# Attention followed by two feed-forward layers in float32: the values of two heads side by side in column halves of the array, their sums by ones in its quarters, and the rotary step on GpSimd

## The chip, the core and the metric

One core of a Trainium2 chip runs the whole program. The metric is the time of one execution on the device, in microseconds. Engines are named as the profile names them: PE (TensorE), PEld (its weight loads), DVE (VectorE), ACT (ScalarE), POOL (GpSimd), SP (the queue that issues every DMA).

## The reference

q, k and v are float32 of 4 batches x 8 heads x 576 positions x 64. Cut to what matters:

```
q_rot, k_rot = (rotate(q), rotate(k))            # x1*cos - x2*sin, x1*sin + x2*cos
scores = scale * np.matmul(q_rot, k_rot.transpose(0, 1, 3, 2))
scores = scores - np.max(scores, axis=-1, keepdims=True)
attn = np.exp(scores)
attn = attn / (np.sum(attn, axis=-1, keepdims=True) + 1e-09)
x = np.matmul(attn, v)                           # then [2304 tokens, 512]
h = x @ w_in;  x = (h - np.tanh(h)) @ w_out      # d_ff = 2048
h = x @ w_in2; x = (h * sigmoid(1.702 * h)) @ w_out2
```

## The kernel before

There are 32 heads in 16 pairs, and a head's 576 positions are 5 tiles of 128 (the last holds 64). The order of all work is written out by hand, engine by engine; semaphores tie the engines together.

For each head the program does this. **Rotary** (`rope`, on DVE, three products and sums over 128 partitions x 576 for the keys of a pair and three for its queries). **Split** into a high and a low part of float32 (`keys_hi` and `queries_hi` on ACT, `keys_lo` and `queries_lo` on DVE), with a DMA copy of the high part to the other 64 partitions (`copy_k`, `copy_q`). **Near scores** (`near_scores`, entry "M" of the ring, L414): two matmuls of 288 columns for a tile of 128 queries, from which DVE takes the rows' maxima (`row_max`, L667). **Maxima across** (`maxima_across`, "R", L421): PE transposes the 5 columns of maxima, and DVE puts them into the rows of the query tile (`place_maxima`, L674). **Scores** (`scores`, "S", L431 and L437): four matmuls for a tile of 128 keys, with the maximum subtracted inside the product, and the exponential on ACT (`exp`, L537). **Values** (`probs_v`, L449): two float32 matmuls of 288 columns with 128 x 128 weights, in which 64 columns are V and 64 columns are ones, so that the sums of the exponentials come out beside the values. ACT copies the result out (`copy_pv`), the sums go through DMA, a reciprocal on DVE (`invert`), a scratch in HBM and a broadcast DMA, and POOL multiplies (`normalise`, L382).

PSUM has 3 slots of two banks for S, M and R, which go round in the order of the list `RING`; an entry waits until the entry 3 places before it has been read. The last two banks belong to the values. PE issues, in a head, S and the values of two tiles before, with the near scores of the next head between them:

```
for t in range(TILES):
    ...
    if now:
        scores(h, t)
    if now and g >= 0:
        probs_v(g)
    if ahead and t < 2:
        near_scores(h + 1, 2 * t + 1)
        near_scores(h + 1, 2 * t + 2)
```

Keys and queries have 4 sets of tiles (`k_hl`, `k_one`, `q_hh`, `q_max`), and are split 3 heads ahead. After the heads come the two feed-forward layers (L485, L500, L503); from head 17 on, the first x tiles and weights for them are cut into high and low parts between the heads' work (`early_x`, `early_w`).

## Time and profile before

| | |
|---|---|
| median of 3 runs | 1146.83 us (1146.66 to 1147.7) |
| the profiled execution | 1147.27 us, of which the span is 1145.5 us |
| PE busy | 1104.1 us, 96% of the span |
| DVE busy | 552.4 us, 48% |
| ACT busy | 425.7 us, 37% |
| POOL busy | 57.1 us, 5% |

Attention takes up the first 341 us of the span or so, the feed-forward layers the rest. The shares are averages over both parts; the rows further down take attention by itself.

### The profile page before, as it was taken

How to read it: one execution, taken by the hardware profiler on the slowest of the kernel's cores; microseconds unless marked ns; L12 is line 12 of the kernel's file. 1: busy time of each engine (PE TensorE's matmuls, PEld its weight loads, DVE VectorE, ACT ScalarE, POOL GpSimd, SP SyncE). 2: the span in 40 equal slices, each digit the busy share in tenths (PEclk: the TensorE clock that was granted, in tenths of full speed). 3: DMA queues.
4: the chain of work that ended last, by engine and by line, in shares of the span. 5: the costliest groups of instructions: out<-in, count | busy, mean ns of one | idle time of the engine just before them, and what ended most of it. 6: DMA issues, size and time to landing. Idle time of an engine off the chain costs nothing.

```text
span 1145.5 us, 15078 instructions
## 1 busy us (share of the span) xinstructions
PE 1104.1 (96%) x5952; PEld 1017.8 (89%) x5952; DVE 552.4 (48%) x879; ACT 425.7 (37%) x747; POOL 57.1 (5%) x62
## 2 busy tenths in 40 slices
PE   2999998999999999999999999999999999999998
PEld 1888877787789999999999999999999999999997
DVE  7888887888736433232233333455232322323222
ACT  2555554555544423222222323445232222323222
POOL 3011111102111000000000000000000000000000
PEclk9999999999999999999999999999999999999999
DMA  6355557566315300000000100062000000000000
GB/s 182 95 158 127 155 154 201 136 169 166 87 61 178 102 28 29 28 28 11 19 28 28 29 28 28 1 193 83 28 28 28 28 1 28 28 28 1 28 1 28
DMA packets 78854, 79.85 MB, mean 70 GB/s; under 512 B 30144, under 2 KB 55744, under 8 KB 78784
## 3 DMA queue, kind: packets, MB, share of 16 engines
q1 hardware_dynamic: 78784, 78.89, 24.1%
q8 instruction: 47, 0.77, 0.3%
q14 instruction: 23, 0.19, 0.1%
HBM read 55.12 MB, written 14.23 MB: 61 GB/s over the span
## 4 chain that ended last, share of the span: by engine, by line
PE 89%; DVE 7%; SPq 1%; DMA 1%; POOL 1%; issue 1%; ACT 0%; POOLq 0%; DVEq 0%; ACTq 0%
PE PS L485 35%; PE PS L503 17%; PE PS L500 17%; PE PS L449 10%; PE PS L414 3%; PE PS L431 3%; PE PS L437 3%; DVE neg_max L667 2%; DVE q_max L684 1%; DVE k_hl L679 1%; DVE q_max L674 1%; DMA turned_k<-k_dram 1%; DVE raw_q L662 0%; DVE w_parts L697 0%; DVE raw_q L660 0%
## 5 line engine op out<-in xcount | busy, mean ns | idle before, releaser
L485 PE MATMUL PS<-x_hi,w_parts 128*128 128x384 f32 x1536 | 423.1, 336 | 0.0
L742 DVE TENSOR_TENSOR g_raw<-PS,act_t 128x384 f32<-128x384 f32 x192 | 107.0, 557 | 400.2 <-ACT act_t L610 202.1
L485 PEld LDWEIGHTS PS<-x_hi,w_parts 128*128 128x128 f32 x1536 | 280.5, 188 | 4.3
L485 PE MATMUL PS<-x_lo,w_parts 128*128 128x384 f32 x768 | 257.2, 335 | 0.0
L500 PE MATMUL PS<-g_hi,w_parts 128*128 128x384 f32 x768 | 210.3, 334 | 0.8 <-DVE g_lo L747 0.8
L503 PE MATMUL PS<-w_parts,g_hi 128*128 128x512 f32 x576 | 195.1, 393 | 1.0 <-DVE y_sb L756 0.8
L449 PE MATMUL PS<-probs,v_one 128*128 128x288 f32 x640 | 183.4, 409 | 0.3 <-ACT pv_sb L545 0.3
L747 DVE TENSOR_TENSOR g_lo<-g_raw,g_hi 128x384 fp32r<-128x384 f32 x192 | 107.7, 561 | 113.6 <-ACT g_hi L617 113.6
L537 ACT ACTIVATE probs<-PS 128x576 f32<-128x576 f32 x160 | 104.0, 650 | 129.6 <-PE PS L437 126.3
L485 PEld LDWEIGHTS PS<-x_lo,w_parts 128*128 128x128 f32 x768 | 144.2, 188 | 4.2
L617 ACT ACTIVATE g_hi<-g_raw 128x384 fp32r<-128x384 f32 x192 | 100.8, 525 | 122.9 <-DVE g_raw L742 119.7
L500 PEld LDWEIGHTS PS<-g_hi,w_parts 128*128 128x128 f32 x768 | 140.0, 188 | 1.1 <-DVE g_lo L747 1.1
L449 PEld LDWEIGHTS PS<-probs,v_one 128*128 128x128 f32 x640 | 112.4, 191 | 18.1 <-issue 0.5
L667 DVE TENSOR_REDUCE neg_max<-PS 128x1 f32<-128x576 f32 x160 | 113.8, 746 | 30.1 <-PE PS L414 29.5
L500 PE MATMUL PS<-g_lo,w_parts 128*128 128x384 f32 x384 | 128.3, 334 | 0.0
L503 PEld LDWEIGHTS PS<-w_parts,g_hi 128*128 128x128 f32 x576 | 108.1, 188 | 21.9 <-issue 1.1
L610 ACT ACTIVATE act_t<-PS 128x384 f32<-128x384 f32 x96 | 47.2, 492 | 212.5 <-PE PS L485 212.5
L608 ACT ACTIVATE act_t<-PS 128x384 f32<-128x384 f32 x96 | 47.2, 492 | 206.9 <-PE PS L485 206.9
L414 PE MATMUL PS<-k_hl,q_hh 128*128 128x288 f32 x320 | 86.7, 376 | 34.8 <-DMA q_hh<-q_hh 17.5
L503 PE MATMUL PS<-w_parts,g_lo 128*128 128x512 f32 x288 | 113.7, 395 | 0.0
L414 PEld LDWEIGHTS PS<-k_hl,q_hh 128*128 128x128 f32 x320 | 56.4, 200 | 51.8 <-issue 19.7
L431 PE MATMUL PS<-q_hh,k_hl 128*128 128x288 f32 x320 | 80.0, 332 | 0.0
(51 smaller groups left out, 741.3 us busy)
## 6 DMA issues: line engine op xcount, KB each, us to landing
x_raw<-x_scratch SPq DMA_DIRECT2D x12, 768.0 KB, 4.5
raw_w<-moe_w_in_dram SPq DMA_DIRECT2D x32, 256.0 KB, 3.1
raw_w<-moe_w_out_dram SPq DMA_DIRECT2D x32, 256.0 KB, 3.3
raw_k<-k_dram SPq DMA_DIRECT2D x16, 288.0 KB, 3.5
turned_k<-k_dram SPq DMA_DIRECT2D x64, 72.0 KB, 3.2
raw_q<-q_dram SPq DMA_DIRECT2D x16, 288.0 KB, 3.8
turned_q<-q_dram SPq DMA_DIRECT2D x64, 72.0 KB, 3.5
k_one<-k_hl SPq DMA_DIRECT2D x32, 144.0 KB, 2.4
```

The costliest lines, as they stand in the source:

```text
L414: last = nc.tensor.matmul(slot[:, b, :], q_hh[h % 4][:, t * P:(t + 1) * P], k_hl[h % 4][:, b * HALF:(b + 1) * HALF], start=True, stop=True)
L431: nc.tensor.matmul(slot[:, b, :], k_hl[h % 4][:, keys], q_hh[h % 4][:, b * HALF:(b + 1) * HALF], start=True, stop=False)
L449: last = nc.tensor.matmul(pv_banks[:, b, :], v_one[h // 2 % 2][:, h % 2, t, :], probs[g % PROBS][:, b * HALF:(b + 1) * HALF], start=t == 0 ...
L485: last = nc.tensor.matmul(h_banks[j % 2], w_parts[j][:, w, c * P:(c + 1) * P], x[par][:, c, :], start=(c == 0 and w == 0 and x is x_hi), s ...
L500: last = nc.tensor.matmul(acc_banks[c][:, 0:UNIT], w_parts[j][:, w, c * P:(c + 1) * P], g[:, s, :], start=start, stop=stop)
L503: last = nc.tensor.matmul(acc_banks[c], g[:, s, c * P:(c + 1) * P], w_parts[j][:, w, :], start=start, stop=stop)
L537: nc.scalar.activation(probs[g % PROBS][:, :].rearrange("p (b n) -> p b n", b=2), slot_halves(slot_of("S", h, t)), ACT.Exp).then_inc(exp_d ...
L608: nc.scalar.activation(act_t[:, j % 2, :], h_banks[j % 2], ACT.Tanh).then_inc(act_done, 1)
L617: nc.scalar.activation(g_hi[:, j % STAGES, :], g_raw[:, j % 2, :], ACT.Copy).then_inc(g_hi_done, 1)
L667: nc.vector.tensor_reduce(neg_max[h % 2][:, t:t + 1], slot_halves(slot_of("M", h, t)), AX.XY, ALU.max, negate=True).then_inc(max_done, 1)
L742: nc.vector.tensor_tensor(g_raw[:, j % 2, :], h_banks[j % 2], act_t[:, j % 2, :], ALU.subtract if m == 0 else ALU.mult).then_inc(g_done, 1)
L747: nc.vector.tensor_tensor(g_lo[:, j % STAGES, :], g_raw[:, j % 2, :], g_hi[:, j % STAGES, :].bitcast(F32), ALU.subtract).then_inc(g_lo_don ...
```

## The change

The unit of attention becomes the pair. **Values** (`values`): for each tile of keys, the V of head a takes 64 columns of the array as weights (columns 0 to 63 for the even head, 64 to 127 for the odd), with that head's exponentials as the moving operand: one matmul of 512 columns and one of 64 for each head. The sums come from four matmuls whose weights are 32 columns of ones, one for each half of 288 positions of each head, written to the four quarters of the partitions. V is laid out on the host in one array with both heads in a row (`value_tiles`), and comes with one DMA. **Order**: in step n of a pair PE issues S of the even head, then near scores, the values of the step before, S of the odd head, and near scores again; `near_plan` says how many. The maxima of both heads are transposed together. **Sets**: keys and queries have 6 sets, of which the last two of `k_hl` and `q_hh` lie in `g_hi` and `g_lo`, and there are 6 tiles of exponentials, of which three lie in `y_sb`. **Rotary**: pair 0 stays on DVE, all the others go to POOL, on which `normalise` is now one product over 128 partitions. The feed-forward layers are as before. The core of the diff:

```
-PROBS = 5
-PV_LAG = 2
-PREPARED = 3
+PROBS = 6
+SETS = 6
+UNITS_PV = PAIRS * TILES
+
+
+def near_plan(pair):
+
+    if pair == 0:
+        return [(0, 0), (0, 2), (2, 2), (2, 2), (0, 0)]
+    return [(1, 2), (1, 2), (1, 1), (1, 1), (0, 0)]
...
+def pair_steps(pair):
+
+    steps, i = [], 0
+    for a, b in near_plan(pair):
+        ahead = near_tiles(pair + 1) if pair + 1 < PAIRS else []
+        steps.append((ahead[i:i + a], ahead[i + a:i + a + b]))
+        i += a + b
+    return steps
...
+    order = [("M", h, t) for h, t in near_tiles(0)] + [("R", 0, 0)]
+    for pair in range(PAIRS):
+        for n, (first, second) in enumerate(pair_steps(pair)):
+            order.append(("S", 2 * pair, n))
+            order += [("M", h, t) for h, t in first]
+            if n == TILES - 1 and pair + 1 < PAIRS:
+                order.append(("R", 2 * pair + 2, 0))
...
-        pv_banks = PS[:, 6:8, 0:HALF]
+        values_wide, values_tail, sum_rows = PS[:, 6, :], PS[:, 7, 0:TAIL], PS[:, 7, TAIL:TAIL + HALF]
...
-        k_one = [sb(f"k_one{j}", [P, PADDED], F32R, one_stack) for j in range(4)]
         q_hh = [sb(f"q_hh{j}", [P, PADDED], F32R, one_stack) for j in range(4)]
-        q_max = [sb(f"q_max{j}", [P, PADDED], F32R, one_stack) for j in range(4)]
-        v_one = [sb(f"v_one{j}", [P, 2, TILES, P], stack=one_stack) for j in range(2)]
-        probs = [sb(f"probs{j}", [P, SEQ], stack=one_stack) for j in range(PROBS)]
+        for tiles, home in ((k_hl, g_hi), (q_hh, g_lo)):
+            tiles += [home.rearrange("p s n -> p (s n)")[:, j * PADDED:(j + 1) * PADDED] for j in range(2)]
+        k_one = [sb(f"k_one{j}", [P, PADDED], F32R, one_stack) for j in range(SETS)]
+        q_max = [sb(f"q_max{j}", [P, PADDED], F32R, one_stack) for j in range(SETS)]
+        v_sb = [sb(f"v_sb{j}", [P, TILES, P], stack=one_stack) for j in range(2)]
+        ones = sb("ones", [P, 2, 32], stack=one_stack)
...
+            def fetch_sums(pair):
+                sp.wait_ge(pv_copied, pair + 1)
                 if pair >= 2:
                     sp.wait_ge(inv_out, 16 * (pair - 1))
-                sp.dma_start(sums[pair % 2][a * HD:(a + 1) * HD, :],
-                             pv_sb[h % 4][row:row + 1, :].rearrange("o (p j) -> o p j", j=SEQ // HD)).then_inc(sums_in[pair % 2], 16)
...
+            for pair in range(PAIRS):
+                if pair:
+                    fetch_sums(pair - 1)
+                if pair + 2 < PAIRS:
+                    copy_k(2 * pair + 4)
+                    copy_q(2 * pair + 4)
+                if pair + 1 < PAIRS:
+                    load_v(pair + 1)
+                if pair >= 2:
+                    store_x(pair - 2)
+                if pair + 2 < PAIRS:
+                    copy_k(2 * pair + 5)
+                    copy_q(2 * pair + 5)
+                if pair:
+                    store_inverse(pair - 1)
+                if pair + 4 < PAIRS:
+                    for t, src in (("k", k_d), ("q", q_d)):
+                        sp.wait_ge(k_lo_done if t == "k" else q_lo_done, 2 * pair + 6)
+                        load(t, src, pair + 4)
+                if pair:
+                    spread_inverse(pair - 1)
...
+            def rope(t, pair):
+                par, at = pair % 2, 3 + 4 * (pair - 1) + (2 if t == "k" else 4)
+                pool.wait_ge(loaded[t][par], (pair // 2 + 1) * 80)
+                nc.gpsimd.tensor_tensor(turned[t][par][:, :], turned[t][par][:, :], sin_sb[:, :], ALU.mult).then_inc(pool_chain, 1)
+                nc.gpsimd.tensor_tensor(raw[t][par][:, :], raw[t][par][:, :], cos_sb[:, :], ALU.mult).then_inc(pool_chain, 1)
+                pool.wait_ge(pool_chain, at)
+                nc.gpsimd.tensor_tensor(raw[t][par][:, :], raw[t][par][:, :], turned[t][par][:, :],
+                                        ALU.add).then_inc(k_roped if t == "k" else q_roped, 1)
 
             def normalise(pair):
-                par = pair % 2
-                pool.wait_ge(inv_in[par], pair // 2 * 32 + 32)
-                pool.wait_ge(pv_copied, 2 * pair + 2)
+                pool.wait_ge(inv_in[pair % 2], pair // 2 * 32 + 32)
+                pool.wait_ge(pv_copied, pair + 1)
+                nc.gpsimd.tensor_tensor(pv_sb[pair % 3][:, :], pv_sb[pair % 3][:, :], inv_wide[pair % 2][:, :],
+                                        ALU.mult).then_inc(norm_done, 1)
+
+            pool.wait_ge(consts_in, 32)
+            for pair in (1, 2):
+                rope("k", pair)
+                rope("q", pair)
...
+            for pair in range(PAIRS):
                 if pair >= 2:
-                    pool.wait_ge(x_stored[par], pair // 2 * 16)
-                for a in range(2):
-                    last = nc.gpsimd.tensor_tensor(x_out[par][own(a), :], pv_sb[(2 * pair + a) % 4][own(a), :],
-                                                   inv_wide[par][own(a), :], ALU.mult)
-                last.then_inc(norm_done, 1)
-                pool.wait_ge(norm_done, pair + 1)
-
-            for pair in range(PAIRS - 1):
-                normalise(pair)
+                    normalise(pair - 2)
+                if pair + 3 < PAIRS:
+                    rope("k", pair + 3)
+                    rope("q", pair + 3)
+            normalise(PAIRS - 2)
...
-            def probs_v(g):
-                h, t = divmod(g, TILES)
-                pe.wait_ge(exp_done, g + 1)
+            def values(unit):
+
+                pair, t = divmod(unit, TILES)
+                pe.wait_ge(exp_done, 2 * unit + 2)
                 if t == 0:
-                    pe.wait_ge(loaded["v"][h // 2 % 2], h // 4 * 64 + 64)
-                    if h:
-                        pe.wait_ge(pv_copied, h)
-                for b in range(2):
-                    last = nc.tensor.matmul(pv_banks[:, b, :], v_one[h // 2 % 2][:, h % 2, t, :],
-                                            probs[g % PROBS][:, b * HALF:(b + 1) * HALF], start=t == 0, stop=t == TILES - 1)
-                last.then_inc(pv_done, 1)
+                    pe.wait_ge(loaded["v"][pair % 2], pair // 2 * 16 + 16)
+                    if pair:
+                        pe.wait_ge(pv_copied, pair)
+                first, last = t == 0, t == TILES - 1
+                p = [probs[(2 * unit + a) % PROBS] for a in range(2)]
+                for bank, cols in ((values_wide, slice(0, BANK)), (values_tail, slice(BANK, SEQ))):
+                    for a in range(2):
+                        nc.tensor.matmul(bank[own(a), :], v_sb[pair % 2][:, t, own(a)], p[a][:, cols],
+                                         start=first, stop=last, skip_group_check=True)
+
+                for g in range(4):
+                    done = nc.tensor.matmul(sum_rows[32 * g:32 * g + 32, :], ones[:, t // FULL, :],
+                                            p[g // 2][:, g % 2 * HALF:(g % 2 + 1) * HALF], start=False, stop=last,
+                                            skip_group_check=True)
+                done.then_inc(pv_done, 1)
...
+            for pair in range(PAIRS):
+                for n, (first, second) in enumerate(pair_steps(pair)):
+                    scores(2 * pair, n)
+                    for h, t in first:
+                        near_scores(h, t)
+                    if pair * TILES + n:
+                        values(pair * TILES + n - 1)
+                    if n == TILES - 1 and pair + 1 < PAIRS:
+                        maxima_across(pair + 1)
+                    scores(2 * pair + 1, n)
+                    for h, t in second:
+                        near_scores(h, t)
...
+            def copy_pv(pair):
+                act.wait_ge(pv_done, (pair + 1) * TILES)
+                if pair >= 3:
+                    act.wait_ge(x_stored[(pair - 3) % 2], (pair - 3) // 2 * 16 + 16)
+                nc.scalar.activation(pv_sb[pair % 3][:, 0:BANK], values_wide, ACT.Copy)
+                nc.scalar.activation(pv_sb[pair % 3][:, BANK:SEQ], values_tail, ACT.Copy)
+                if pair >= 2:
+                    act.wait_ge(sums_in[pair % 2], pair // 2 * 64)
+                nc.scalar.activation(sum_sb[pair % 2][:, :], sum_rows, ACT.Copy).then_inc(pv_copied, 1)
...
+            for pair in range(PAIRS):
+                a, b = 2 * pair + 4, 2 * pair + 5
+                for n in range(TILES):
+                    exp(2 * pair, n)
+                    if n == 0 and pair:
+                        copy_pv(pair - 1)
+                    exp(2 * pair + 1, n)
+                    if pair == 0:
+                        if n == 0:
+                            for h in range(2, 4):
+                                keys_hi(h)
+                                queries_hi(h)
+                        if n == 3:
+                            keys_hi(4)
+                        if n == 4:
+                            queries_hi(4)
+                            keys_hi(5)
+                            queries_hi(5)
+                    elif b < NHEADS:
+                        if n == 1:
+                            keys_hi(a)
+                            queries_hi(a)
+                        if n == 2:
+                            keys_hi(b)
+                        if n == 3:
+                            queries_hi(b)
...
+            for h in range(2):
+                split(h)
+            for h, t in near_tiles(0):
+                row_max(h, t)
+            for h in range(2):
+                place_maxima(h)
+            for pair in range(PAIRS):
+                a, b = 2 * pair + 4, 2 * pair + 5
+                for n, (first, second) in enumerate(pair_steps(pair)):
+                    if pair == 0 and n == 0:
+                        split(2)
+                        split(3)
+                    for h, t in first + second:
+                        row_max(h, t)
+                    if pair and b < NHEADS and n == 1:
+                        split(a)
+                    if pair and b < NHEADS and n == 3:
+                        split(b)
+                    if n == 3 and pair:
+                        invert(pair - 1)
+                    if n == TILES - 1 and pair + 1 < PAIRS:
+                        for h in (2 * pair + 2, 2 * pair + 3):
+                            place_maxima(h)
...```

The row of PE for two steps of a head, before (L414 near scores, L431 and L437 scores, L449 values, L421 the transpose of the maxima):

```order
L414 MATMUL PS<-k_hl,q_hh 128x288 x4
L431 MATMUL PS<-q_hh,k_hl 128x288 x2
L437 MATMUL PS<-q_max,k_one 128x288 x2
L449 MATMUL PS<-probs,v_one 128x288 x2
L421 MATMUL PS<-ident,neg_max 5x128
```

And after, for one step of a pair and the beginning of the next (L468 and L474 scores, L449 near scores, L490 values, L494 sums):

```order
L468 MATMUL PS<-q_hh,k_hl 128x288 x2
L474 MATMUL PS<-q_max,k_one 128x288 x2
L449 MATMUL PS<-k_hl,q_hh 128x288 x2
L490 MATMUL PS<-probs,v_sb 64x512 x2
L490 MATMUL PS<-probs,v_sb 64x64 x2
L494 MATMUL PS<-probs,ones 32x288 x4
L468 MATMUL PS<-q_hh,k_hl 128x288 x2
L474 MATMUL PS<-q_max,k_one 128x288 x2
L449 MATMUL PS<-k_hl,q_hh 128x288 x4
```

Two matmuls of 288 columns with full weights, for one head, have become eight narrow ones for both heads, which stand between the scores of the even and of the odd head.

The row of DVE for one head in the middle of attention, before (L667 row maxima, L659 to L662 rotary, L674 placing the maxima, L679 and L684 low parts):

```order
L667 TENSOR_REDUCE neg_max<-PS 128x1 x4
L659 TENSOR_TENSOR turned_q<-turned_q,sin_sb 128x576
L660 TENSOR_TENSOR raw_q<-raw_q,cos_sb 128x576
L662 TENSOR_TENSOR raw_q<-raw_q,turned_q 128x576
L674 TENSOR_TENSOR q_max<-PS,g_raw 5x640
L679 TENSOR_TENSOR k_hl<-raw_k,k_hl 64x576
L684 SCALAR_TENSOR_TENSOR q_max<-raw_q,q_hh 64x576
```

And after, for one pair (L737, L744, L749 and L754 are the same works, L761 and L763 the inversion):

```order
L737 TENSOR_REDUCE neg_max<-PS 128x1 x6
L749 TENSOR_TENSOR k_hl<-raw_k,k_hl 64x576
L754 SCALAR_TENSOR_TENSOR q_max<-raw_q,q_hh 64x576
L737 TENSOR_REDUCE neg_max<-PS 128x1 x4
L749 TENSOR_TENSOR k_hl<-raw_k,k_hl 64x576
L754 SCALAR_TENSOR_TENSOR q_max<-raw_q,q_hh 64x576
L761 TENSOR_SCALAR sums<-sums 128x9
L763 RECIPROCAL sums<-sums 128x9
L744 TENSOR_TENSOR q_max<-PS,g_raw 5x640 x2
```

The rotary step has left the row, and the second split and the inversion of a pair now stand directly ahead of the placing of the maxima.

The row of POOL for one pair, after (before it held only two products of `normalise`, 64x576 each):

```order
L410 TENSOR_TENSOR pv_sb<-pv_sb,inv_wide 128x576
L401 TENSOR_TENSOR turned_k<-turned_k,sin_sb 128x576
L402 TENSOR_TENSOR raw_k<-raw_k,cos_sb 128x576
L404 TENSOR_TENSOR raw_k<-raw_k,turned_k 128x576
L401 TENSOR_TENSOR turned_q<-turned_q,sin_sb 128x576
L402 TENSOR_TENSOR raw_q<-raw_q,cos_sb 128x576
L404 TENSOR_TENSOR raw_q<-raw_q,turned_q 128x576
```

Seven products stand there for a pair, and the first of them waits for the broadcast of an inverse.

## Rows read from the trace of the kernel before

**Rows 1.** The page: the span and the busy time of each engine.

```profile
span 1145.5 us, 15078 instructions
PE 1104.1 (96%) x5952; PEld 1017.8 (89%) x5952; DVE 552.4 (48%) x879; ACT 425.7 (37%) x747; POOL 57.1 (5%) x62
```

**Rows 2.** Busy time in stretches: length, PE, PEld, DVE, ACT, POOL, PEclk, DMA share, GB/s.

```profile
60.00:100.00 40.00, 39.93 (x226) 33.99 (x225) 35.53 (x54) 23.00 (x36) 5.63 (x4) 1.00 0.59 158
100.00:200.00 100.00, 94.11 (x515) 79.14 (x514) 85.70 (x124) 53.69 (x84) 15.71 (x10) 0.98 0.62 163
200.00:300.00 100.00, 94.30 (x523) 79.31 (x521) 88.62 (x127) 56.90 (x88) 18.23 (x12) 1.00 0.56 147
```

**Rows 3.** One line, L449: durations min/median/max in ns, first and last start.

```profile
L449 PE MATMUL PS<-probs,v_one x640: 403/406/687, 32.5 to 340.1; 128*128 128x288 f32 x160
```

**Rows 4.** Timeline of PE: start us, us from first start to last end, instructions.

```profile
202.26 0.43 PE L431 MATMUL PS<-q_hh,k_hl 128*128 128x288 f32 x2
202.53 0.43 PE L437 MATMUL PS<-q_max,k_one 69*128 69x288 f32 x2
202.79 1.14 PE L449 MATMUL PS<-probs,v_one 128*128 128x288 f32 x4
...
204.29 0.43 PE L431 MATMUL PS<-q_hh,k_hl 128*128 128x288 f32 x2
...
204.83 1.14 PE L449 MATMUL PS<-probs,v_one 128*128 128x288 f32 x4
205.81 0.27 PE L421 MATMUL PS<-ident,neg_max 128*5 128x128 f32 x1
205.84 0.51 PE L431 MATMUL PS<-q_hh,k_hl 128*128 128x288 f32 x2
206.18 0.43 PE L437 MATMUL PS<-q_max,k_one 69*128 69x288 f32 x2
```

**Rows 5.** Timeline of POOL: start, length, idle time before and its releaser.

```profile
103.42 2.87 POOL L382 TENSOR_TENSOR x_out<-pv_sb,inv_wide 64x576 f32<-64x576 f32 x2 [15.42 <-DMA inv_wide<-inv_scratch]
121.55 2.87 POOL L382 TENSOR_TENSOR x_out<-pv_sb,inv_wide 64x576 f32<-64x576 f32 x2 [15.26 <-DMA inv_wide<-inv_scratch]
139.76 2.87 POOL L382 TENSOR_TENSOR x_out<-pv_sb,inv_wide 64x576 f32<-64x576 f32 x2 [15.34 <-DMA inv_wide<-inv_scratch]
...
203.83 2.89 POOL L382 TENSOR_TENSOR x_out<-pv_sb,inv_wide 64x576 f32<-64x576 f32 x2 [14.45 <-issue]
```

**Rows 6.** Groups of DVE by shape, attention: busy us, mean ns, idle before.

```profile
L667 DVE TENSOR_REDUCE neg_max<-PS 128x1 f32<-128x576 f32 x160 | 113.8, 746 | 30.1 <-PE PS L414 29.5
L674 DVE TENSOR_TENSOR q_max<-PS,g_raw 5x640 fp32r<-5x640 f32 x32 | 25.9, 811 | 2.9 <-PE PS L421 2.5
L684 DVE SCALAR_TENSOR_TENSOR q_max<-raw_q,q_hh 64x576 fp32r<-64x576 f32 x32 | 25.2, 788 | 5.6 <-ACT q_hh L557 4.6
L660 DVE TENSOR_TENSOR raw_q<-raw_q,cos_sb 128x576 f32<-128x576 f32 x16 | 12.0, 751 | 0.0
```

**Rows 7.** Timeline of ACT and DVE near 203 to 207 us.

```profile
202.99 0.65 ACT L537 ACTIVATE probs<-PS 128x576 f32<-128x576 f32 x1 [1.41 <-PE PS L437]
...
204.23 1.42 DVE L667 TENSOR_REDUCE neg_max<-PS 128x1 f32<-128x576 f32 x2 [0.64 <-PE PS L414]
205.57 1.76 DVE L659 TENSOR_TENSOR turned_k<-turned_k,sin_sb 128x576 f32<-128x576 f32 x1
```

**Rows 8.** Timeline of the start.

```profile
4.44 0.59 DVE L708 MEMSET k_one<- 5x640 f32 x1 [4.44 <-POOL q_hh L369]
...
6.31 0.42 SPq L201 DMA_DIRECT2D raw_k<-k_dram  x1
...
8.39 0.59 DVE L708 MEMSET k_one<- 5x640 f32 x1 [0.73 <-POOL q_hh L369]
...
14.23 0.68 ACT L557 ACTIVATE q_hh<-raw_q 64x576 fp32r<-64x576 f32 x1 [1.38 <-DVE raw_q L662]
...
17.46 1.78 PE L414 MATMUL PS<-k_hl,q_hh 128*128 128x288 f32 x6 [17.46 <-DMA q_hh<-q_hh]
...
23.82 0.68 PE L431 MATMUL PS<-q_hh,k_hl 128*128 128x288 f32 x2
```

305 lines of the change are left out of this document (123 added, 182 removed).

## The prediction

> **What bounds the kernel now.** I read the page first: PE is busy for 96% of the span, and no other engine for half of it [rows 1]. The change touches attention alone, so I cut that out by stretches: between 60 and 300 us PE is busy for 94 to 100% and DVE for 86 to 89%, with the clock at 0.98 to 1.00, that is the level of 2.4 GHz nearly all the time [rows 2]. So there are two engines near their limit, and a cut of either alone is soon stopped by the other. Then I took the pace. POOL multiplies once in a pair, at 103.42, 121.55 and 139.76 us: 18.1 to 18.2 us for a pair [rows 5]. PE's timeline gives its parts. Four scores matmuls (L431, L437) take from 202.26 to 202.79, 0.53 us. The values of a tile take from 204.83 to 205.81, where L421 starts: 0.98 us in four records, since every float32 matmul is two, so 0.245 us for a record of 288 columns. Between 202.79 + 0.98 and 204.29 lie two near-score tiles, 0.26 us each. The transpose takes 0.11 us (206.18 less two times 0.13 is 205.92, against 205.81) [rows 4]. A pair is then 10 x 0.98 + 10 x 0.53 + 10 x 0.26 + 0.2 = 17.9 us. The pace of 18.1 is PE's own sum: in the quiet pairs PE waits for nobody, and what shortens the values shortens the pair until another wait opens. Over all of attention the mean is worse: from the first to the last L449, 32.5 to 340.1 us, it is 307.6 / 16 = 19.2 us [rows 3], since later pairs also carry cuts of x and weights, and some pairs stall.
>
> **What the change takes off PE.** The cost is in columns streamed. For a tile of both heads it was 4 x 288 = 1152 columns in full width, 1.96 us. Now there are 2 x 512 + 2 x 64 + 4 x 288 = 2304 columns, but in halves and quarters of the array. At the rate of [rows 4] a record of 512 columns is 0.436 us, one of 64 is 0.054, one of 288 is 0.245, each twice. Everything hangs on whether matmuls in different columns run at the same time; no row of this trace shows it. From above, none of it overlaps: 2 x (2 x 0.436 + 2 x 0.054 + 4 x 0.245) = 3.92 us. From below all of it does: 2 x (0.436 + 0.054 + 0.245) = 1.47 us. I take the lower bound, 1.5 us, as likeliest, because the narrow tiles share neither columns nor partitions of the output, and these are the resources that a matmul of full width holds.
>
> The only narrow matmul before is the transpose with 5 columns of weights. It starts 0.98 us after its predecessors and the next full matmul streams 0.11 us behind it, for 128 columns in two passes (2 x 128 / 288 x 0.12 = 0.11): going from full to narrow and back costs nothing to be seen [rows 4]. The Trainium skill, TensorEngine Tiling (Array Packing), Key Properties, says that a change of tiling mode drains TensorE. By that page there would be three drains in each tile's work, 240 in attention; the row shows none, so I add nothing.
>
> PE's sum for a pair is 5 x 1.5 + 5.3 + 2.6 + 0.2 = 15.6 us, 2.3 less.
>
> **What it takes off DVE and puts on POOL.** DVE loses six products of 0.75 us per pair, 4.5 us. It keeps 10 x 0.746 of maxima, 2 x 0.811 of placing, 4 x 0.75 of low parts and 0.4 of inversion: 12.5 us [rows 6]. POOL gets seven products. One of 64 x 576 takes 1.44 us (2.87 for two) [rows 5]; for 128 partitions nothing says more, since every partition holds the same 576 elements. From above, twice that would be 20 us and would bind; I take 1.44, so 10.1 us.
>
> They don't add freely. POOL ran from 203.83 to 206.72; the row maxima on DVE at 204.23 took 1.42 for two, as ever, but the product at 205.57 took 1.76 instead of 0.75 us, and so ended 0.6 us after POOL did [rows 5, 7]. So a DVE product with two inputs in SBUF waits for a POOL product to end; one that reads PSUM does not. With POOL busy for 10 of some 18 us, each of the four low parts meets it with a chance of 0.55 and then loses 1.0 us: 2.2 us per pair on DVE, 14.7 in all. DVE does not bind by its sum, only by place.
>
> **Where PE will wait.** The order is new, and with three slots in the ring each place has to be looked at.
> - S of the even head in step 1 takes the slot of S of the odd head in step 0. ACT reads that only after the three copies of `copy_pv`, which start when the values before it end. 576 columns take ACT 0.65 us [rows 7]; 864 in three pieces are 0.98 to 1.95, I take 1.25. With 0.2 to start and 0.65 for the exponential, the slot is free 2.15 us after the values, and PE has 0.53 + 0.52 to do: a wait of 1.1.
> - The same in step 2 without the copies: the exponential ends 0.85 us after the scores (202.79 to 203.64) [rows 4, 7], and two near-score tiles cover 0.52. A wait of 0.4 (with the signals).
> - At the pair's end DVE has, behind the last near scores: a maximum, two low parts, the inversion and two placings, 0.85 + 1.5 + 0.4 + 0.8 + 0.8 = 4.4 us. PE has scores, values, transposes, scores and half a scores tile, 0.53 + 1.5 + 0.22 + 0.53 + 0.27 = 3.05, waits for the first placing (3.6) and then at the next near score for the second (4.4). 1.1 in sum. Before, a head's placing was followed by two tiles of other work.
> - The lock between DVE and POOL adds 0 to 2.2; since DVE is idle for 4 of 18 us, most delays end in its own gaps, and I take 0.4.
>
> The pair is 15.6 + 1.1 + 0.4 + 1.1 + 0.4 = 18.6 us. The gain in matmuls is 2.3, and 3.0 of new waits stand against it; what is won is the difference to the 19.2 of the mean, because keys are now split two pairs ahead and a late DMA should not reach PE.
>
> **The start.** POOL clears six sets, 1.32 us each (4.44 to 8.39 for three), so DVE is free at 8.39 + 0.59 + 2.6 = 11.6. Then it does six rotary products for pair 0 while POOL, whose loads were issued from 6.31 on, does six for pair 1: one waits for the other, 0.75 + 5 x (1.44 + 0.75) = 11.7, until 23.3. ACT needs 0.68, and the copy and its signal 17.46 - 14.91 = 2.55: the first near scores at 26.5 instead of 17.46 [rows 8]. Ten maxima, a transpose and a placing take 8.9: the first scores at 35.5 instead of 23.82 (28 if the lock does not bite). In pair 0, four low parts against POOL's six products stand ahead of the maxima of pair 1: 4 us more.
>
> **The sum.** Attention ends at 35.5 + 4 + 16 x 18.6 - 2.6 (the last pair has no near scores) = 334.5 us, instead of 340.5. Cuts of x and weights, and the last pairs without splits, I let cancel. The feed-forward part has the same instructions and stays. The profiled execution took 1147.3, of which the span was 1145.5; its successor takes 1141.3, and against the median, 0.4 lower, I say 1141.
>
> **The rivals.**
> 1. *The waits eat it.* Halves run together, but the lock falls on the pair's end each time (2.2 instead of 0.4): 20.4 us per pair, 363 us, 1170. The breakeven is at (340.5 - 36.9) / 16 = 19.0 us, 0.4 above my sum. For it: DVE's last chain is in the shadow of nothing. Against it: POOL's products start only when the inverse of two pairs before is back.
> 2. *Matmuls start in order, and a float32 matmul is two.* The low record of head a must wait for its own high record in the same columns, and head b's high record cannot pass it; so high a, low a with high b, low b: three lengths in place of two, and five in place of two for the quarters. Values cost 3 x 0.436 + 2 x 0.054 + 5 x 0.245 = 2.64 us, more than 1.96. PE's sum is 21.3, with waits of 1.5 in front of steps 1 and 2 22.8 us: 402 us, 1208. This is the case on the other side, and it decides from values of about 1.95 us on. What speaks for it: in [rows 4] equal records follow each other at 0.245 us with none starting early. The Trainium skill, TensorE: Matmul & The Clock Gate, Part 3, says that matmuls of different tiles overlap, but that they start and end strictly in program order; taken to the letter, with two records per tile, that is this rival. No row here has two tiles at once to bear it out.
> 3. *No overlap.* 3.92 us, 29.2 per pair, 504 us, 1310. Against it: nothing but that disjoint columns have no reason to wait.
> 4. *A clean gain.* No lock, shorter copies: 17 us per pair, a start at 28: 302 us, 1108. It is the good end of the first case.
>
> **How the numbers follow.** The halves run together with 0.68: gain 0.45, within 0.2% (about what a measurement of this kernel can tell from no change) 0.07, slower by rival 1 0.16. Rival 2 has 0.22, rival 3 0.10. So faster 0.45, same 0.07, slower 0.48: the two signs are near even, and the likeliest single case is a small gain, with a range of its own of 1112 to 1170. The range for all has to reach over about half of rival 2: 1112 to 1208.
>
> **What would show it.** Right: L490 and L494 take 1.5 us from the first start to the next L468; the pair's pace (one L410 to the next) is 17.5 to 19.5 us; PE waits for ACT in front of L468 in step 1, and for L744 at the pair's end; DVE's L749 and L754 are often 1.8 us. Wrong: values of 2.6 us (rival 2) or 3.9 (rival 3); products of 128 partitions on POOL of over 2 us; a first L468 at 28 us instead of 35.

## The result and the profile after

The changed kernel takes 1203.28 us (median of 4 runs, 1202.2 to 1205.74), the one before 1146.74 us on the same chip (1146.3 to 1147.7): a ratio of 1.0495, 95% interval 1.0477 to 1.0513. The prediction said 1141 us in a range of 1112 to 1208. The time lies inside the range only because the range was stretched towards the 1208 of rival 2. No part of rival 2 is true, as the rows will show, so that is luck.

First the page of the kernel after, span and busy times. It answers to [rows 1].

```profile
span 1200.4 us, 16265 instructions
PE 1123.7 (94%) x6592; PEld 955.3 (80%) x6592; DVE 524.1 (44%) x790; ACT 417.9 (35%) x763; POOL 175.1 (15%) x138
```

The three engines did what the edit says: DVE lost 28 us, POOL gained 118. Yet the share of "busy PE" hardly moved, and does not show the loss. The stretches do (length; PE, PEld, DVE, ACT, POOL; granted clock; DMA share; GB/s), against [rows 2]:

```profile
60.00:100.00 40.00, 35.20 (x249) 20.42 (x246) 23.34 (x28) 16.55 (x29) 18.56 (x12) 0.93 0.46 119
100.00:200.00 100.00, 86.96 (x637) 52.29 (x637) 64.24 (x82) 44.77 (x78) 45.04 (x29) 0.98 0.47 121
200.00:300.00 100.00, 86.23 (x620) 51.91 (x620) 67.43 (x82) 45.34 (x79) 48.43 (x30) 0.97 0.57 150
```

In attention PE is busy for 87 of 100 us instead of 94, DVE for 64 instead of 86. Both engines now wait: neither is the bound by its sum. The clock is that of the 2.4 GHz level most of the time, but less so than before, and that costs something too (further down). The line of the values, to set beside [rows 3]:

```profile
L490 PE MATMUL PS<-probs,v_sb x324: 219/454/1117, 36.6 to 393.7; 128*64 128x512 f32 x81, 128*64 128x64 f32 x81
```

From the first value to the last it is 357.1 us, or 22.3 for a pair; it was 307.6, or 19.2. That is 49.5 us; 4.1 more come from the later first value (36.6 instead of 32.5). Together they are 53.6 of the 54.9 us between the two spans. So nearly all of it is in attention.

**One block of values.** PE's timeline, the values of one tile pair and what stands around them:

```profile
181.90 0.43 PE L449 MATMUL PS<-k_hl,q_hh 128*128 128x288 f32 x2
182.26 0.64 PE L490 MATMUL PS<-probs,v_sb 128*64 128x512 f32 x1
182.26 0.64 PE L490 MATMUL PS<-y_sb,v_sb 128*64 128x512 f32 x1
...
182.74 0.59 PE L490 MATMUL PS<-probs,v_sb 128*64 128x512 f32 x1
...
182.75 0.59 PE L490 MATMUL PS<-y_sb,v_sb 128*64 128x512 f32 x1
...
183.17 0.22 PE L490 MATMUL PS<-probs,v_sb 128*64 128x64 f32 x1
...
183.22 0.22 PE L490 MATMUL PS<-probs,v_sb 128*64 128x64 f32 x1
...
183.38 0.44 PE L494 MATMUL PS<-probs,ones 128*32 128x288 f32 x2
...
183.65 0.41 PE L494 MATMUL PS<-probs,ones 128*32 128x288 f32 x2
...
184.00 0.53 PE L468 MATMUL PS<-q_hh,k_hl 128*128 128x288 f32 x2
...
184.38 0.42 PE L474 MATMUL PS<-q_max,k_one 128*128 128x288 f32 x2
```

Heads a (`probs`) and b (`y_sb`) start together, record by record: the high record of both at 182.26, the low one of both at 182.74. Halves and quarters do run at the same time, and the two records of a float32 matmul don't get in the way. This refutes rivals 2 and 3. But there is a gap at every change of the tile's size. The two L449 records last to 182.16 (0.26 for two, as in [rows 4]), and L490 starts at 182.26. The last L490 record of 64 columns (0.055) ends at 183.28, and L494 starts at 183.38. The last L494 record (0.25) ends at 183.90, and L468 starts at 184.00. Three times 0.10 us. Behind the last one, L468 takes 0.38 up to L474 instead of 0.26, another 0.12. From L449's start to L474's start it is 184.38 - 181.90 = 2.48 us. With full-width values the same stretch is 2 x 0.98 + 2 x 0.26 = 2.48 [rows 4]. The gain in columns, 1.96 - 1.54 = 0.42 us in a block, is given back in full at the changes of size.

**The wait for a row maximum.** Engines other than PE, just behind that block:

```profile
181.92 1.41 POOL L401 TENSOR_TENSOR turned_k<-turned_k,sin_sb 128x576 f32<-128x576 f32 x1
...
182.29 1.66 DVE L749 TENSOR_TENSOR g_hi<-raw_k,g_hi 64x576 fp32r<-64x576 f32 x1
...
183.29 1.94 POOL L402 TENSOR_TENSOR raw_k<-raw_k,cos_sb 128x576 f32<-128x576 f32 x1
...
183.98 1.86 DVE L754 SCALAR_TENSOR_TENSOR q_max<-raw_q,g_lo 64x576 fp32r<-64x576 f32 x1
...
185.31 1.80 POOL L404 TENSOR_TENSOR raw_k<-raw_k,turned_k 128x576 f32<-128x576 f32 x1
...
185.77 1.40 DVE L737 TENSOR_REDUCE neg_max<-PS 128x1 f32<-128x576 f32 x2
...
186.56 0.53 PE L468 MATMUL PS<-q_hh,k_hl 128*128 128x288 f32 x2 [1.50 <-DVE neg_max L737]
```

Low parts (L749, L754) and POOL's products take turns: each waits for the other's whole instruction, so a low part costs 1.66 and 1.86 instead of 0.75, and POOL's product 1.94 and 1.80 instead of 1.41. The maximum, which reads PSUM, runs beside POOL at 0.70. But it stands behind both low parts, 3.5 us of DVE, and PE stands still for 1.5 us until a slot is read.

PE's waits over attention (what it waited for: us in total, times, longest):

```profile
PE PS L449 <- DMA q_hh<-q_hh: 23.6, 1, 23.6
PE PS L468 <- DVE neg_max L737: 14.2, 12, 1.8
PE PS L474 <- DVE q_max L744: 13.3, 14, 2.3
PE PS L468 <- ACT y_sb L582: 6.4, 20, 0.4
PE PS L449 <- DVE q_max L744: 3.3, 13, 0.3
```

The pair that begins at 181.3 takes 21.9 us: PE's sum of 17.9 and 4.1 of waits, namely 1.67 for this maximum, 0.63 and 0.41 for the two placings, 0.59 behind the copies, and two of 0.38 for an exponential. (I count from the end of streaming, so 0.1 or 0.2 more than the rows' idle time.)

**What the waits do to the clock.** One pair later the same wait takes 1.81 us, and behind it PE does not run at its full speed:

```profile
208.78 0.83 PE L468 MATMUL PS<-q_hh,k_hl 128*128 128x288 f32 x2 [1.81 <-DVE neg_max L737]
```

```profile
208.00:210.00 2.00, 1.22 (x5) 1.22 (x6) 1.40 (x3) 0.10 (x1) 2.00 (x2) 0.71 0.82 275
210.00:212.00 2.00, 2.00 (x7) 0.75 (x7) 0.76 (x1) 0.65 (x1) 2.00 (x2) 0.50 0.00 0
```

A granted clock of 0.50 is the 1.2 GHz level: from this L468 to its L474 it is 0.63 us (208.78 to 209.41) where the pair before took 0.37. The mean granted clock of the profiled execution is 0.991, against 0.997 before and 0.999 in the run splits_apart below. If PE streams all through the low stretches, as it does in this one, they cost (1 - 0.991) x 1200 = 11 us here, 3 before and 1 or 2 in splits_apart. These are estimates, worked out from the mean clocks. No run changed the clock by itself, and all that is said below of waits includes what follows them in this way.

### The profile page after: what moved, and what is told of

Read it like the earlier page. It is cut to its first block, busy times and chain, and to the rows that moved or that the text cites. A ratio compares the mean times of both kernels' runs of the same rounds, so it can differ in the third digit from the quotient of the medians.

```text
span 1200.4 us, 16265 instructions
## 1 busy us (share of the span) xinstructions
PE 1123.7 (94%) x6592; PEld 955.3 (80%) x6592; DVE 524.1 (44%) x790; ACT 417.9 (35%) x763; POOL 175.1 (15%) x138
## 3 DMA queue, kind: packets, MB, share of 16 engines
q1 hardware_dynamic: 62144, 79.41, 23.1%
HBM read 55.64 MB, written 14.23 MB: 58 GB/s over the span
## 4 chain that ended last, share of the span: by engine, by line
PE 82%; DVE 13%; ACT 2%; issue 2%; POOL 1%; DMA 0%; SPq 0%; POOLq 0%; DVEq 0%; ACTq 0%
PE PS L531 33%; PE PS L549 17%; PE PS L546 16%; PE PS L490 6%; DVE neg_max L737 4%; DVE q_max L754 3%; PE PS L494 3%; PE PS L468 3%; PE PS L449 2%; DVE k_hl L749 2%; DVE q_max L744 2%; PE PS L474 2%; ACT y_sb L582 1%; DVE g_hi L749 1%; ACT probs L582 0%
## 5 line engine op out<-in xcount | busy, mean ns | idle before, releaser
L737 DVE TENSOR_REDUCE neg_max<-PS 128x1 f32<-128x576 f32 x160 | 115.9, 752 | 112.4 <-PE PS L449 112.1
L549 PE MATMUL PS<-w_parts,g_lo 128*128 128x512 f32 x288 | 113.8, 395 | 0.0
L582 ACT ACTIVATE y_sb<-PS 128x576 f32<-128x576 f32 x79 | 51.4, 652 | 95.5 <-PE PS L474 95.2
L474 PE MATMUL PS<-q_max,k_one 69*128 69x288 f32 (+1 forms) x320 | 70.7, 303 | 13.5 <-DVE q_max L744 13.3
L582 ACT ACTIVATE probs<-PS 128x576 f32<-128x576 f32 x81 | 52.4, 649 | 76.4 <-PE PS L474 76.0
L449 PE MATMUL PS<-k_hl,q_hh 128*128 128x288 f32 x220 | 48.2, 323 | 27.8 <-DMA q_hh<-q_hh 23.6
L546 PEld LDWEIGHTS PS<-g_lo,w_parts 128*128 128x128 f32 x384 | 72.1, 188 | 0.0
L468 PE MATMUL PS<-q_hh,k_hl 128*128 128x288 f32 x220 | 56.9, 341 | 15.3 <-DVE neg_max L737 9.6
```

What stands on the lines that cost most here:

```text
L449: last = nc.tensor.matmul(slot[:, b, :], q_hh[h % SETS][:, t * P:(t + 1) * P], k_hl[h % SETS][:, b * HALF:(b + 1) * HALF], start=True, sto ...
L468: nc.tensor.matmul(slot[:, b, :], k_hl[h % SETS][:, keys], q_hh[h % SETS][:, b * HALF:(b + 1) * HALF], start=True, stop=False)
L474: last = nc.tensor.matmul(slot[:, b, :], k_one[h % SETS][rows, keys], q_max[h % SETS][rows, b * HALF:(b + 1) * HALF], start=False, stop=True)
L546: last = nc.tensor.matmul(acc_banks[c][:, 0:UNIT], w_parts[j][:, w, c * P:(c + 1) * P], g[:, s, :], start=start, stop=stop)
L549: last = nc.tensor.matmul(acc_banks[c], g[:, s, c * P:(c + 1) * P], w_parts[j][:, w, :], start=start, stop=stop)
L582: nc.scalar.activation(probs[i % PROBS].rearrange("p (b n) -> p b n", b=2), slot_halves(slot_of("S", h, t)), ACT.Exp).then_inc(exp_done, 1)
```

## The experiments

Theory A from here on: (1) narrow values gain nothing on PE, since three changes of size eat the columns saved; (2) the low parts, shut out by POOL, stand ahead of maxima that PE waits for; (3) the start is later. The table has medians of 4 or 5 runs with an interval, or a single run ("one run"), by which a difference of a few us is not shown. The kernel before took 1146.7 to 1148.6 beside them. "Last value" is the start of the last matmul of the values.

| run | us | ratio to before | last value |
|---|---|---|---|
| before | 1146.7 | 1 | 340.1 |
| after | 1203.3 | 1.0495 [1.0477, 1.0513] | 393.7 |
| no_rotary | 1170.0 | one run | 361.6 |
| rotary_on_dve | 1196.8 | 1.0417 [1.0391, 1.0442] | 386.4 |
| splits_apart | 1174.7 | 1.0230 [1.0198, 1.0262] | 364.7 |
| splits_apart_rotary_dve | 1190.7 | 1.0360 [1.0343, 1.0377] | 383.1 |
| full_width | 1205.5 | one run | 397.7 |
| sums_in_halves | 1196.3 | one run | 387.7 |
| sums_between | 1204.4 | one run | 396.2 |
| full_width_apart | 1192.7 | 1.0395 [1.0378, 1.0413] | 384.6 |
| full_halves_apart | 1181.0 | 1.0294 [1.0278, 1.0309] | 371.9 |
| sums_in_halves_apart | 1167.2 | 1.0179 [1.0161, 1.0197] | 356.4 |
| values_in_twos | 1176.5 | 1.0256 [1.0235, 1.0277] | 370.5 |
| late_rotary | 1173.4 | 1.0228 [1.0213, 1.0244] | 365.1 |
| queries_on_pool | 1193.3 | 1.0385 [1.0363, 1.0408] | 385.2 |
| store_late | 1142.6 | 0.9961 [0.9945, 0.9977] | 333.9 |

### Who shuts out the maxima

**no_rotary.** POOL's two products and sum per tensor become one sum of a single column.

```diff
-                nc.gpsimd.tensor_tensor(turned[t][par][:, :], ..., sin_sb[:, :], ALU.mult)
-                nc.gpsimd.tensor_tensor(raw[t][par][:, :], ..., cos_sb[:, :], ALU.mult)
-                nc.gpsimd.tensor_tensor(raw[t][par][:, :], ..., turned[t][par][:, :], ALU.add)
+                nc.gpsimd.tensor_tensor(raw[t][par][:, 0:1], ..., turned[t][par][:, 0:1], ALU.add)
```

> Leaves out the rotary step of pairs 1 to 15: POOL only adds one column of each tile. Theory A (in the changed kernel a pair takes 21.9 us, of which PE streams or switches tiles for 17.9 and waits for 4.1; about 1.7 of the waits, and a good part of the late start, come from DVE and POOL shutting each other out of SBUF): the low parts on DVE fall from up to 1.9 us back to 0.75, the wait before the scores of step 3 falls from 1.7 to under 0.3, the first scores come some 8 us earlier, a pair takes 20.2 to 20.6 us and the whole 1165 to 1175 us. Theory B (the waits come from the order of work and the three slots alone, and DVE only happens to be slow where PE waits anyway): pair 21.5 us or more, time 1190 or more.

1170.0 us: without POOL's rotary 33 us go, of some 56. Where PE still waits:

```profile
PE PS L471 <- DVE q_max L741: 5.9, 14, 0.4
...
PE PS L465 <- DVE neg_max L734: 1.7, 4, 0.6
```

The maxima are down from 14.2 us to 1.7, the first placing from 13.3 to 5.9. The first matmul behind the placed maxima (L471, L474 in the kernel after) comes at 28.8 instead of 33.9. So the rotary work on POOL is behind most of the loss, whether by its lock or by its length, and 23 us stay even without any.

**rotary_on_dve.** Rotary of all pairs back on DVE (two `rope` calls of three instructions per pair, ahead of the second group of maxima).

> The rotary step of all pairs is back on DVE, in the gaps between the first and the second near scores of steps 2 and 3; everything else as changed. Theory A: DVE carries 4.5 us more per pair (17 of 20) but nothing is shut out; pair 20 to 21 us, time 1160 to 1180 us, faster than the changed kernel by 2 to 3.5%. Theory B: DVE's sum grows and the order is as it was, so the pair grows to 22.5 or more and the time to 1205 or more.

1196.8 us, a miss. No lock, but DVE has 4.5 us more per pair, and they stand ahead of the maxima too: PE waits for the placing 20.7 us in 15 times, 1.4 each. The lock is one way to make DVE late; work of its own at the same place is another, and costs almost as much. (The clock is low here as well, 0.987 to 0.989 in the four runs.)

**splits_apart.** The same low parts, one at a time instead of two together: two of them between the first and the second maxima of a step, one behind the maxima, and the one of the odd head's queries behind the placing, with the inversion.

```diff
-                    for h, t in first + second:
+                    for h, t in first:
+                        row_max(h, t)
+                    if pair and b < NHEADS and n == 2:
+                        queries_lo(a)
+                    if pair and b < NHEADS and n == 3:
+                        keys_lo(b)
+                    for h, t in second:
                         row_max(h, t)
                     if pair and b < NHEADS and n == 1:
-                        split(a)
-                    if pair and b < NHEADS and n == 3:
-                        split(b)
-                    if n == 3 and pair:
-                        invert(pair - 1)
+                        keys_lo(a)
...
+                    if n == TILES - 1 and pair and b < NHEADS:
+                        queries_lo(b)
+                    if n == TILES - 1 and pair:
+                        invert(pair - 1)
```

> Rotary stays on POOL; on DVE the two low parts of a head are taken apart and put where no maxima stand right behind them, and the second query part and the inversion go behind the placing of the maxima. Theory A: the wait of 1.7 in step 3 falls to 0.3, those for the placing of the maxima from 1.0 to 0.3; pair 19.6 to 20.2 us, time 1165 to 1175 us. Theory B' (PE is held by the ring and by ACT, DVE's order matters little): pair above 21 us, time above 1190.

1174.7 us, 29 less with not one instruction fewer: point (2) is shown, with the inversion's move in the same edit. By the mean clocks (0.996 to 0.999 in its four runs, 0.988 to 0.991 in those of the kernel after) some 7 to 10 of the 29 come by way of the clock, an estimate. The wait for a maximum before L468 is nearly gone (1.0 us in all instead of 14.2; 6.5 us in 10 times come up before L449), and a quiet pair takes 20.0. The lock itself is not gone. Between 40 and 345 us a low part takes 0.96 us in the mean instead of 1.26, but the first instruction of the inversion (L761) takes 1.10 instead of 0.17: what meets POOL now is work that PE does not wait for. Some pairs still stall. Rows of one, with SP's:

```profile
217.41 0.60 SPq L241 DMA_DIRECT2D q_hh<-q_hh  x1
...
218.63 1.66 DVE L744 TENSOR_TENSOR q_max<-PS,g_raw 5x640 fp32r<-5x640 f32 x2 [0.95 <-PE PS L458]
...
220.93 0.50 PE L449 MATMUL PS<-k_hl,q_hh 128*128 128x288 f32 x2 [0.84 <-DVE q_max L744]
```

The view puts PE's wait down to the placings, but they end at 220.29, 0.64 us before L449 starts; in a quiet pair L449 follows at once (placings to 99.85, L449 at 99.90, wait 0.25). This L449 also needs the copy of the queries, which SP issues at 217.41, and copies of q_hh take 3.4 to 3.8 us to land here. So it is most likely this copy, late in SP's queue, that PE waits for.

**splits_apart_rotary_dve.** Both edits.

> The low parts apart as in the run before, and the rotary step on DVE in the gaps of steps 2 and 3. If the lock between DVE and POOL is what is left of the waits, the pair falls from 20.0 to 19.5 us and the time to 1160 to 1168 us; if DVE's own sum (17 of 20 us) now holds the maxima up, as in the run with the rotary on DVE alone, the pair stays at 21 to 22 us and the time at 1185 to 1195 us. I expect the second, since the rotary products stand between near scores and their maxima.

1190.7 us, the second of the two cases named: with the low parts out of the way, POOL is the better place for the rotary by 16 us. The assignment of the change was right; its order on DVE was not.

### What narrow values are worth

**full_width.** The kernel after with one matmul per head over both heads' V, 8 records in 512 + 64 columns. The two heads are added into one place, and the sums are left out.

```diff
-                        nc.tensor.matmul(bank[own(a), :], v_sb[pair % 2][:, t, own(a)], p[a][:, cols],
+                        nc.tensor.matmul(bank, v_sb[pair % 2][:, t, :], p[a][:, cols],
```

> Values as full-width matmuls in the order of the changed kernel: for each head one of 512 and one of 64 columns with 128 columns of weights (the V of both heads), no separate sums. Both heads are added into the same place and the sums are copied from the values, so the numbers are not the reference's; the columns streamed are those of the kernel before (1152 a tile and pair). Theory A (the narrow form costs 1.95 us from the last full matmul to the next full one, 1.56 of streaming and 0.4 of changes between tile sizes, so as much as the 1.96 of the full form): the values take 1.96 us, pair and time stay within 0.5% of the changed kernel's 1203. Theory C (the narrow form is in itself a gain or a loss, and the changes of tile size are hidden): over 1% off.

1205.5 us, no difference that a single run can tell. I took that for point (1). **full_width_apart** was to repeat it where PE binds more (the same edit on splits_apart).

> The kernel with the low parts taken apart (1174.7 us, 20.0 us a pair), with its values as full-width matmuls of 512 and 64 columns and no separate sums, as in the earlier run on the changed kernel; both heads are added into one place and the sums are copied from the values, so the numbers are not the reference's. Here few waits are left that could hide a difference on PE. Theory A (narrow form 1.95 us a block, full form 1.96): the pair stays at 20.0 and the time within 0.5% of 1174.7 us. Theory C (the narrow form is worth something, and in the changed kernel its waits hid it): the full form is slower by over 8 us.

1192.7 us: 18 more than splits_apart, against my theory. In the order of the kernel after, something had hidden a difference: there full_width waits 3.7 us for placings instead of 13.3 and 10.3 for maxima instead of 14.2, and its mean clock is 0.999 instead of 0.991, some 10 us by the estimate above. The block:

```profile
216.00 0.43 PE L449 MATMUL PS<-k_hl,q_hh 128*128 128x288 f32 x2
216.26 1.02 PE L490 MATMUL PS<-probs,v_sb 128*128 128x512 f32 x2
217.12 1.02 PE L490 MATMUL PS<-y_sb,v_sb 128*128 128x512 f32 x2
217.97 0.33 PE L490 MATMUL PS<-probs,v_sb 128*128 128x64 f32 x2
218.14 0.39 PE L490 MATMUL PS<-y_sb,v_sb 128*128 128x64 f32 x2
218.34 0.51 PE L468 MATMUL PS<-g_lo,g_hi 128*128 128x288 f32 x2
218.69 0.42 PE L474 MATMUL PS<-q_max,k_one 128*128 128x288 f32 x2
```

The four records of 64 columns take 0.37 us (217.97 to 218.34) where their columns need 0.22, and L468 is slow too: 2.69 us from L449 to L474 instead of 2.48. So this comparison had a flaw of its own, the 512 + 64 split at full width. The next run shows its price: 11.7 us of the 18 go with the split.

**full_halves_apart.** The same with 288 + 288 columns, as the kernel before has them.

```diff
-                for bank, cols in ((values_wide, slice(0, BANK)), (values_tail, slice(BANK, SEQ))):
+                for bank, cols in ((PS[:, 6, 0:HALF], slice(0, HALF)), (PS[:, 7, 0:HALF], slice(HALF, SEQ))):
```

> The kernel with low parts apart and the values at full width again, but in column halves of 288 + 288 instead of 512 + 64 (one matmul for each head, tile and half, 8 records in a block; V of the two heads is accumulated together, and the sums are left out, so values and sums are wrong; the three copies take 288 columns each). The run with full width in 512 + 64 took 1192.7 us, 18 above the kernel with narrow values, and its timeline shows the four records of 64 columns 0.11 us apart instead of 0.055, after which the next near score also starts late. Theory A (the narrow values save nothing against a proper full width; it was the 64-column records, too short to hide the weights' load, that cost the 18 us): a block of 1.96 us from the first L490 to the next L468, a pace near 20.0 us, and 1170 to 1180 us. Rival B (narrow values do save some 0.2 us in a block, whatever the split of the columns): blocks of 2.1 us again and 1186 to 1196 us. Rival C (the ACT copies decide, which are 864 columns in three here as there): within 3 us of 1192.7 with blocks of 1.96.

```profile
212.20 0.43 PE L449 MATMUL PS<-k_hl,q_hh 128*128 128x288 f32 x2
212.46 2.10 PE L490 MATMUL PS<-y_sb,v_sb 128*128 128x288 f32 x8
214.19 0.64 PE L468 MATMUL PS<-g_lo,g_hi 128*128 128x288 f32 x2
214.66 0.42 PE L474 MATMUL PS<-q_max,k_one 128*128 128x288 f32 x2
```

2.46 us from L449 to L474: the block is as long as the narrow one (2.48), as point (1) says. The kernel takes 1181.0 us, just over my 1170 to 1180, and 6.3 more than the narrow one. Rival B and rival C are out. A quiet pair takes 20.5 instead of 20.0, and its rows show where. One part is in step 1, from L474 to the next L468: 1.55 us (205.72 to 207.27) against 1.38 in splits_apart (223.47 to 224.85). The narrow form's last change of size comes after the values are done, so ACT starts the copies 0.23 us before L474 instead of 0.06 (223.24 against 223.47; 205.66 against 205.72). The other part is the fifth block, which the transposes follow: from the last L474 to L458 it is 2.42 us (116.78 to 119.20) against 2.12 in splits_apart (115.76 to 117.88). Behind that block the 0.12 of the way back is not paid, and the first change of size falls into a gap that the full-width form has too. So narrow values gain nothing in four blocks of five, and 0.3 us in the fifth; 0.17 and 0.30 us in a pair account for the 6 us.

**sums_in_halves, sums_between, sums_in_halves_apart.** In the first the sums are two matmuls with 64 columns of ones in the halves (one change of size fewer; the first 288 columns alone are summed, the rest is left out). In the second L490's tail, the sums and L490's wide part follow each other (one change more, same work). The third is the first on splits_apart.

> The changed kernel with the four sums matmuls (32 columns of ones) replaced by two of 64 columns, for the first 288 positions of each head; the sums of the other positions are left out. The columns streamed at one time are the same (288, twice), and the array stays in halves from the values to the sums. Theory A (a change of tile size costs 0.10 us wherever it stands, and 0.20 on the way back to full width, where the weights' load shows too): the gap of 0.10 between the last value matmul and the first sums matmul is gone, the others stay; the block from the last full matmul to the next takes 1.85 instead of 1.95 us, the whole 1193 to 1200 us. Theory D (the gap is a wait for the exponentials or for issuing many short instructions, not for the tile size): the gap stays at 0.10 and so does the time, 1203.

> The same matmuls as the changed kernel in another order: the 64-column values, the sums, then the 512-column values, so that there are four changes of tile size in a block instead of three. Theory A: one more gap of 0.10 us, the block takes 2.05, the whole 1205 to 1212 us. Theory D: no more gap, 1203 us.

> The kernel with low parts apart, the sums taken by 64 columns of ones in the array's halves (the first 288 columns alone are summed, so the sums are wrong): one change of tile size fewer in a block, 0.10 us. If each change of tile size lies on the path, 80 blocks give 8 us less: 1163 to 1170 us, a pace of 19.5. If waits refill the gap, 1172 to 1176 us.

The third one's rows, and then those of sums_between:

```profile
206.00 1.19 PE L490 MATMUL PS<-probs,v_sb 128*64 128x512 f32 x8
207.03 0.66 PE L494 MATMUL PS<-probs,ones 128*64 128x288 f32 x4
207.61 0.54 PE L468 MATMUL PS<-g_lo,g_hi 128*128 128x288 f32 x2
```

```profile
205.25 0.69 PE L496 MATMUL PS<-probs,ones 128*32 128x288 f32 x8
205.87 1.08 PE L490 MATMUL PS<-probs,v_sb 128*64 128x512 f32 x4
206.88 0.53 PE L468 MATMUL PS<-q_hh,k_hl 128*128 128x288 f32 x2
```

L490 to L494 is 1.03 us where it was 1.12 in the block of the kernel after: with both at 64 columns of weights the gap is gone. In sums_between, from the sums to the next L490 it is 0.62 as it was to L468 (0.49 of columns), so 64 to 32 and back costs about 0.1 in each direction. In time: 1196.3, that is 7.0 less than after, and 1204.4, under my 1205 to 1212 and within the spread of the kernel after; each is one run, and the second shows nothing by its time. The third takes 1167.2 against 1174.7. Spread over 80 blocks these 7.5 us are 0.094 each, but that it comes out so even is in part luck: quiet pairs take 19.3 instead of 20.0, 0.7 less where five changes of size are 0.5, and stalled pairs (one of 23.6) take some of it back. So in the good order this change of size is on the path at its full price.

**values_in_twos.** On splits_apart, values of two tiles at a time, so that there are three blocks in a pair instead of five and 6 changes of size fewer.

> On top of the low parts taken apart: the values of two steps in one block (values of both, then sums of both), so 3 blocks in a pair instead of 5 and 6 changes of tile size fewer. Theory A: 2 x 0.4 = 0.8 us per pair less on PE, 13 us in all, if nothing else opens: 1162 us. But in the steps without values, PE has only scores and near scores between two uses of a slot, and should wait for ACT and DVE there: I expect 0.5 to 1.5 us of new waits per pair, so 1165 to 1185 us.

1176.5 us, no gain: PE's sum falls (a quiet pair takes 19.7 instead of 20.0), but a double block comes later (the first value at 44.2 instead of 36.6), and new waits for ACT open in front of L449 (3.7 us in 6 times, up to 2.7). What is saved in changes is lost in coarser steps: one pair takes 27.1 us, and pair 0 25.0 instead of 21.3. (The profiled run is the slowest of the four, with a mean clock of 0.990; the others have 0.994 to 0.997.)

### The start, and rotary before the change

**late_rotary.** On splits_apart, POOL starts its rotary after DVE's low parts of pair 0 (`pool.wait_ge(q_lo_done, 2)`).

> On top of the low parts taken apart: POOL begins its rotary products only when DVE has done the rotary step and the low parts of pair 0. Theory A (the start is late by the lock): first near scores at 19 instead of 23.6 us, first scores at 29 instead of 33.9; but the keys of pair 1 come later by some 5 us, and pair 0 may wait for them. 1168 to 1172 us if they do not show, 1175 if they do; against 1174.7 without it.

1173.4 us, the same as without (1174.7). The first L474 comes at 28.7 instead of 33.9, and then pair 0 takes 26.0 us instead of 21.3. PE waits 1.7 us there for a low part of pair 1's keys, whose rotary was put off, and behind this the granted clock is 0.56 and 0.58 from 38 to 42 and from 42 to 46 us, where splits_apart has 1.00. About 7 us at the 1.2 GHz level cost some 3.4 of the 4.7, an estimate. So the run does not show that the start can't be made shorter; it shows that a wait elsewhere, and the clock behind it, ate what was won.

**queries_on_pool.** The kernel before, with the queries' rotary (pairs 2 to 15) on POOL and nothing else.

> One part of the change alone, in the kernel before: the rotary step of the queries of pairs 2 to 15 goes to POOL, all else stays (heads one by one, full-width values, four sets). Theory A: DVE loses 2.25 us per pair and waits for POOL now and then; in the first pairs, which run at PE's own 18.1 us, nothing is won; in the later ones, with cuts of x and weights on DVE (19.3 us), up to 1 us per pair comes back: 1138 to 1147 us. Rival: the lock hits row maxima's successors in the first pairs too and POOL's chain is late, 1150 to 1165 us.

1193.3 us, the largest miss: 45 us above the 1148.6 beside it for moving three instructions of a pair (with a mean clock of 0.986 to 0.988, so some 12 of them by the estimate above). POOL and DVE at one place (with the idle time before and its releaser):

```profile
214.32 1.40 POOL L392 TENSOR_TENSOR turned_q<-turned_q,sin_sb 128x576 f32<-128x576 f32 x1 [21.55 <-DMA turned_q<-q_dram]
214.99 1.35 DVE L697 TENSOR_TENSOR k_hl<-raw_k,k_hl 64x576 fp32r<-64x576 f32 x1
...
215.68 1.92 POOL L393 TENSOR_TENSOR raw_q<-raw_q,cos_sb 128x576 f32<-128x576 f32 x1
216.36 1.85 DVE L702 SCALAR_TENSOR_TENSOR q_max<-raw_q,q_hh 64x576 fp32r<-64x576 f32 x1
217.68 1.80 POOL L395 TENSOR_TENSOR raw_q<-raw_q,turned_q 128x576 f32<-128x576 f32 x1
```

POOL waits 21.55 us for its load, then needs 5.2 us where DVE needed 2.2, and the split of the next head waits for it. I read this as a loop of load, rotary, split and load with only two tiles; no run had more tiles to show it. One head takes 21.0 us and another 18.1, where others take 9.0. The changed kernel has six sets, splits two pairs ahead, and its view names only two waits of PE for a copy of keys or queries, 23.6 us at the start and 2.8 us at 58.4. That part of the change does what it says, apart from stalls that the view puts down to DVE, as the one in splits_apart.

**store_late.** The kernel before; on SP the store of x stands behind the copies and loads of the step, and the weights' loads are spread over heads 14 to 17.

```diff
-                if h >= 4 and h % 2 == 0:
-                    store_x(h // 2 - 2)
...
                     store_inverse(h // 2 - 1)
+                if h >= 4 and h % 2 == 0:
+                    store_x(h // 2 - 2)
-                if h == 14:
-                    for c in range(STAGING):
-                        load_w(0, c)
+                if 14 <= h < 14 + STAGING:
+                    load_w(0, h - 14)
```

> The kernel before, with two changes on SP's queue alone: the store of the normalised x stands behind the copies and loads of its step instead of in front of them, and the first four weight loads are spread over four heads. Nothing of the change under study is in it. Theory: the 1.1 us per pair by which the mean of the kernel before lies above PE's own 17.9 to 18.1 us is in good part stalls behind SP (it waits for x_out up to 7.1 us with all copies behind it), not DVE's work; then 5 to 12 us go: 1135 to 1142 us. Rival: the stalls are DVE's cuts of x and weights, and the time stays at 1147.

1142.6 us, ratio 0.9961 [0.9945, 0.9977]: faster than both kernels, if only by 0.4%, and 4.8 us where I expected 5 to 12. The kernel before had one head of 15.4 us (transposes at 181.4 and 196.8) with this wait in it:

```profile
192.77 1.51 PE L414 MATMUL PS<-k_hl,q_hh 128*128 128x288 f32 x4 [1.79 <-DVE neg_max L667]
```

The maxima stood behind an inversion that had waited 2.8 us for the DMA of the sums, and behind the wait the clock fell to the 1.2 GHz level: L431 and L437 start 0.48 us apart (194.08, 194.56) instead of 0.27. With the edit this head takes 10.4 us, and the last value starts 6.2 us sooner. From 60 to 340 us its clock is 1.00 in each stretch, where the kernel before has 0.96 to 1.00, so up to 3 us of the gain are the clock's. Which of the two edits did it was not separated; both take work out of the way of the loads on SP.

## Why the prediction was wrong

Its end of attention was 334.5 us; the last value of the kernel after starts at 393.7. By its own steps:

- **Halves run at the same time.** Right, and rivals 2 and 3 fall (head b's high record starts with head a's): L490 and L494 take 1.02 + 0.52 us of columns, 1.54 against my 1.5, rival 2's 2.64 and rival 3's 3.92.
- **"Going from full to narrow and back costs nothing to be seen", so "I add nothing".** This step failed. I judged by the transpose, whose weights have 5 columns. It counts as full width. The kernel after shows it: L458 follows L494 with the gap of 0.10, and no gap stands between it and L468. The changes cost 0.42 us in a block (with 0.04 for the columns, 2.3 in a pair), which is the gain that I had counted: PE's sum is 17.9, not 15.6 (a little less, by the fifth block). Over 16 pairs that is up to 37 of the 59 us missed. The Trainium skill, TensorEngine Tiling (Array Packing), Key Properties, says that a change of mode drains TensorE; the trace agrees, with 0.10 us at each change and 0.12 more behind the way back. It gives no price, but it was right and my row was read wrongly.
- **The wait behind the copies, 1.1.** 0.59; the copies take 0.89 (223.24 to 224.13 in splits_apart), not 1.25 (and my terms add up to 2.1, not 2.15). **Step 2, 0.4.** 0.38, but in two steps of the pair. **The placing, 1.1.** 0.63 + 0.41 = 1.04, right.
- **The lock between DVE and POOL.** This step failed too: the mechanism was right, and its place and what of it reaches PE were wrong. Low parts that met POOL went to 1.66 to 1.98 us, and in the mean a low part took 1.26 between 40 and 345 us, which is 2.0 us more per pair on DVE against my 2.2. Of these I took 0.4 for PE, because "most delays end in its own gaps". In fact two low parts stand in a row ahead of maxima that hold slots, and 1.67 us reach PE. splits_apart gives 29 us back, by order alone. I had looked at this for the pair's end only (rival 1, with 2.2 there and 1170 us), not for step 3, and had no mechanism with waits and a lost gain together.
- **POOL's product of 128 partitions.** 1.41 us against 1.44: right.
- **The start.** First near scores at 23.6 against 26.5, the first L468 at 32.8 against 35.5: about 3 us sooner than I said, since not all six products of DVE met POOL. Pairs 0 and 1 take 21.3 and 25.4 (transposes at 32.5, 53.8, 79.2), where the kernel before had 38.1 for both: 8.6 more, against my 4. Pair 1 has the wait of 2.8 us for a copy in it.
- **The clock.** I carried the 0.98 to 1.00 of before over without a term. The mean of the execution fell from 0.997 to 0.991, an estimated 7 us.
- **The mean of 19.2 as the measure.** A quiet pair of the kernel before took 18.1, so even my own 18.6 was a loss there, and the whole gain hung on stalls going away. The stalls of the kernel before that I hoped the deeper splits would remove were in part SP's queue; store_late removes the largest with two edits.

By the transposes, the 53.6 us at the last value are 9.5 by the first transpose (32.5 instead of 23.1), 8.6 by pairs 0 and 1, and 37.8 by the 13 pairs behind them (22.5 us each instead of 19.6), less 2.3 in the last pair. The order of the low parts (splits_apart) takes 29.0 of them away, 27.6 in the 13 pairs. late_rotary could not shorten the start and pair 0 together. What splits_apart leaves in the 13 pairs is 10.2 us, 0.8 in each. There PE's sum is the old one, and waits for exponentials, maxima and placings, some 2 us in a pair, stand where a quiet pair before had next to none. Their cause, both heads in lockstep with three slots, was argued from the rows and not tried.

## What to carry to other kernels

Before packing matmuls into halves of the array, count the changes of tile size: here one cost 0.10 us and the way back 0.2, so a block of two sizes had to save over 0.4 us to be worth anything. Tiles of one size (sums in halves) were shorter here by one change, though that run takes only half of the sums. When work moves to POOL, look not at DVE's sum but at what stands behind DVE's instructions with two operands in SBUF: put the instruction that another engine waits for ahead of the one that can be shut out. An ablation in a kernel whose waits hide the difference can say "same" where there is one; repeat it where the engine binds. And read the granted clock beside every wait: behind a wait of 1.8 us the matmuls took nearly twice their time (0.63 us for 0.37).

## What was not expected of the hardware

- The price of a change of tile size: 0.10 us from 128 to 64, 64 to 32, 32 to 64, 32 to 128 and 64 to 128 columns of weights, and 0.12 more for the first full-width matmul behind it, but not where a transpose with 5 columns comes first (2.12 us from L474 to L458).
- A float32 matmul's two records of one half pair up with those of the other half; 8 L490 records take 1.03 us.
- At full width four records of 64 columns take 0.37 us instead of the 0.22 of their columns, with weight loads of 128 columns between them; narrow ones of 64 columns follow each other in 0.05 to 0.06 us (183.17, 183.22).
- DVE instructions with two inputs in SBUF and POOL's products waited for each other's end, and both paid: 0.75 becomes up to 1.98 us, 1.41 becomes 1.8 to 2.0, once 2.30. A maximum or a placing, which reads PSUM, stays at 0.70 to 0.81. The Trainium skill, GPSIMD Engine Reference, Specifications, names this contention for DVE instructions with two inputs in SBUF; the trace agrees, and adds the prices. That the price is paid by whatever stands behind on DVE was the surprise.
- POOL takes 1.41 us for 576 columns on 128 partitions, against 1.44 on 64 [rows 5].
- In six places of the kernel after, behind waits of 1.5 to 2.8 us, the granted clock was at the 1.2 GHz level for a while (0.50 at 210 us); the kernel before has two such places, splits_apart one. Not every such wait has one behind it (the 1.50 us at 186.56 has none). So a wait of PE can cost more than its own length.
